# Moving the q and k loads behind the first head's one-hot copies in the SyncE queue, with the preparation steps shifted by one

## The reference

```
q_bits = einsum(q, proj) > 0 ; k_bits = einsum(k, proj) > 0          # 6 bits a row
mask   = bucket(q_bits)[:, :, :, None] == bucket(k_bits)[:, :, None, :]
scores = where(mask, q @ k.T / sqrt(D), -1e9)
attn   = exp(scores - max) / (sum + 1e-9)
x      = (attn @ v) as 1536 tokens x 512
h = x @ w_in1 ; g = (a0 + a1 h + a2 h^2 + a3 h^3) / (1 + |b0||h| + |b1|h^2 + 1e-6) ; x = g @ w_out1
h = x @ w_in2 ; g = h - tanh(h) ; out = g @ w_out2
```

## Time and profile before

| | us |
|---|---|
| median of 3 runs (750.47 to 751.36) | 751.3 |
| the profiled execution's own time | 751.21 |
| its span, first to last instruction | 749.4 |
| outside the span | 1.8 |
| attention, by PE's timeline | up to about 227 |

### The profile page before, as it was taken

How to read it: one execution, slowest core, us unless ns; L and a number is a source line. 1 busy time by engine, 2 the same in 40 slices (tenths; PEclk the granted TensorE clock), 3 DMA queues, 4 the chain that set the end, 5 groups by cost and what they waited for, 6 DMA issues and landing times.

```text
span 749.4 us, 11868 instructions
## 1 busy us (share of the span) xinstructions
PE 734.7 (98%) x3715; PEld 624.8 (83%) x3715; DVE 605.0 (81%) x931; ACT 484.1 (65%) x938; POOL 272.5 (36%) x249
## 2 busy tenths in 40 slices
PE   7998999999999999999999999999999999999998
PEld 4997998998998888788888888888888788888886
DVE  5987998888997999999988888975685698875622
ACT  7887888988897878788766867755553233322321
POOL 6685566566569000000000000000058499992000
PEclk9999999999999999999999999999999999999999
DMA  6758668768745500000000032320000110000101
GB/s 200 176 154 200 186 165 196 192 165 197 165 124 157 188 1 0 1 1 1 1 1 14 30 113 84 111 88 14 1 1 28 43 43 28 15 15 0 57 1 56
DMA packets 43612, 60.21 MB, mean 80 GB/s; under 512 B 7088, under 2 KB 25776, under 8 KB 43568
## 3 DMA queue, kind: packets, MB, share of 16 engines
q1 hardware_dynamic: 43424, 59.26, 29.3%
q10 hardware_dynamic: 144, 0.39, 0.1%
HBM read 31.66 MB, written 3.19 MB: 47 GB/s over the span
## 4 chain that ended last, share of the span: by engine, by line
PE 72%; DVE 10%; SPq 6%; POOL 5%; issue 4%; DMA 3%; ACT 1%; POOLq 0%; ACTq 0%; DVEq 0%
PE acc L867 31%; PE h_ps L833 18%; PE h_ps L957 9%; PE slot L266 5%; PE turn_ps L378 4%; PE pv_ps L342 2%; PE pv_ps L344 2%; DMA kA<-k_hot 2%; SPq L1388 2%; DVE sqr L1155 1%; DVE pol L1176 1%; SPq L1390 1%; DVE pol L1162 1%; SPq L1386 1%; DVE pol L1187 1%
## 5 line engine op out<-in xcount | busy, mean ns | idle before, releaser
L780 POOL TENSOR_TENSOR wout_raw<-win_hi 128x256 f32<-128x256 f32 x8 | 8.9, 1137 | 319.6 <-DVE win_lo L1208 309.2
L608 DVE TENSOR_TENSOR pt_lo<-turn_ps,pt_hi 128x384 fp32r<-128x384 f32 x192 | 97.8, 552 | 16.9 <-ACT pt_hi L522 16.6
L522 ACT ACTIVATE pt_hi<-turn_ps 128x384 fp32r<-128x384 f32 x192 | 85.2, 495 | 26.6 <-PE turn_ps L378 26.1
L833 PE MATMUL h_ps<-x_hi,win_lo 128*128 128x512 f32 x256 | 99.9, 390 | 0.0
L833 PE MATMUL h_ps<-x_lo,win_hi 128*128 128x512 f32 x256 | 99.6, 389 | 0.0
L833 PE MATMUL h_ps<-x_hi,win_hi 128*128 128x512 f32 x256 | 99.6, 389 | 0.0
L566 DVE TENSOR_REDUCE row_min<-slot 128x1 f32<-128x768 f32 x96 | 90.9, 948 | 5.8 <-PE slot L266 5.3
L996 ACT ACTIVATE g_hi<-pol 128x512 fp32r<-128x512 f32 x80 | 50.9, 637 | 66.5 <-PE acc L867 34.1
L454 ACT ACTIVATE E<-slot,row_min 128x768 f32<-128x768 f32 x96 | 87.4, 911 | 2.0 <-issue 1.7
L1200 DVE TENSOR_TENSOR g_lo<-pol,g_hi 128x512 fp32r<-128x512 f32 x80 | 65.9, 824 | 21.7 <-ACT g_hi L996 21.4
L378 PE MATMUL turn_ps<-ident,E 128*128 128x128 f32 x576 | 80.6, 274 | 0.4 <-DVE pt_lo L608 0.3
(11 more groups left out here) (192 smaller groups left out, 1811.4 us busy)
## 6 DMA issues: line engine op xcount, KB each, us to landing
win_raw<-in_moe_w_in SPq DMA_DIRECT2D x32, 256.0 KB, 3.3
wout_raw<-in_moe_w_out SPq DMA_DIRECT2D x32, 256.0 KB, 2.8
v_nat<-in_v SPq DMA_DIRECT2D x8, 384.0 KB, 4.1
q_t<-in_q SPq DMA_DIRECT2D x7, 384.0 KB, 3.1
k_t<-in_k SPq DMA_DIRECT2D x7, 384.0 KB, 3.7
qA<-q_hi SPq DMA_DIRECT2D x14, 192.0 KB, 3.7
qB<-q_hi SPq DMA_DIRECT2D x14, 192.0 KB, 4.0
qB<-q_lo SPq DMA_DIRECT2D x14, 192.0 KB, 4.1
```

The costliest lines, as they stand in the source:

```text
L522: eng.activation(pt_hi[:, c % 2, k0:k0 + T // 2, i * P:(i + 1) * P], turn_ps[h][:, 0:HALF].rearrange("r (k n) -> r k n", n=P), ACT.Copy).t ...
L608: eng.tensor_tensor(pt_lo[dst], turn_ps[h][:, 0:HALF].rearrange("r (k n) -> r k n", n=P), pt_hi[dst].bitcast(F32), ALU.subtract).then_inc( ...
L833: mm = eng.matmul(h_ps[t % 4][:, :], w[:, ws], columns(x, kt, c), start=kt + n == 0, stop=kt == KT - 1 and n == 2)
```

## The change

In SyncE's queue the loads of q and k of pair p + 2 go from the head of each pair's list to a place behind the one-hot copies of head 0 and the load of v, ahead of the split copies of head 1. The dots are taken in step 0 and the one-hots in steps 1 to 4 (they were in 1, and 2 to 5; in the first pair each is one step later than in the others). The sum of head 0 is taken in step 5 on ACT (it was 4), its reciprocal in step 6 on DVE (it was 5), and ACT scales q in step 9 (it was 8).

```diff
-        DOT_STEP = 1
-        HOT_STEPS = {2: (0, 0), 3: (1, 0), 4: (0, 1), 5: (1, 1)}
+        DOT_STEP = 0
+        HOT_STEPS = {1: (0, 0), 2: (1, 0), 3: (0, 1), 4: (1, 1)}
...
-                if first and n == 2:
-                    pe_dots(eng, 1)
-                if prepare and not first and n == DOT_STEP:
+                if prepare and n - first == DOT_STEP:
                     pe_dots(eng, p + 1)
...
-                if turn and n == 8:
+                if turn and n == 9:
                     act_scale(eng, p + 2)
...
-                if n in (4, 9 if last else 11):
+                if n in (5, 9 if last else 11):
                     act_sum(eng, p, n // T)
...
-                if n in (5, 9 if last else 11):
-                    dve_scale(eng, p, n // T)
+                if n in (6, 9 if last else 11):
+                    dve_scale(eng, p, int(n > T))
...
-                if first and n == 2:
-                    dve_bits(eng, 1)
-                if prepare and not first and n == DOT_STEP:
+                if prepare and n - first == DOT_STEP:
                     dve_bits(eng, p + 1)
...
                 def sync_att(p, turn=True):
-                    if turn:
-                        load_qk(p + 2, 0)
-                        load_qk(p + 2, 1)
                     copy_split(p + 1, 0)
                     if not is_zero(p):
                         shift(p - 1, 1)
                     scale_out(p, 0)
                     copy_hot(p + 1, 0)
                     load_v(p + 1)
+                    if turn:
+                        load_qk(p + 2, 0)
+                        load_qk(p + 2, 1)
                     copy_split(p + 1, 1)
```

## The result

The changed kernel takes 772.1 us (median of 5 runs, 769.8 to 776.2) against 751.4 us of the kernel before on the same chip: a ratio of 1.027, 95% interval 1.024 to 1.031, some 20.7 us slower. The profiled execution is the slowest of the five, 776.15 us with a span of 774.3, so that its terms add up to 4 us more than the median.

The account below looks back on a forecast made before the run. PE was taken to bound the kernel, busy 734.7 of 749.4 us. Idle time removed, new waits for q and slow clock sum as 751.2 - 7.1 + 15.8 + 4.4 = 764.3, so 764 us was predicted, range 752 to 773.

Parts of the forecast that it names:

- ACT waits for q in step 9 of six pairs, and PE in step 10: Pairs 0 to 5: q lands 4.3 us after issue, PE waits 2.64 us each, 15.8 us in all.
- v's situation: In SyncE's queue, q with v ahead and copies behind was likened to v, which landed in 4.4 and 5.1 us.
- The clock: Behind PE's new gaps: half of six lower the clock, 3 x 1.47 = 4.4 us lost to slow matmuls.
- the 7.1: PE idle time the change could remove in attention: 5.0 of copy waits, 1.47 of slow matmuls, 2 x 0.29 of scaling.
- The waits removed: PE's step 9 waits for head 0's last one-hot copy, 5.0 us in four places, go or nearly.
- The loop stays hidden: POOL, SyncE's queue and DMA: next q split 1.8 us later, hidden by a pair 2.6 us longer; otherwise next to bind.
- k at nothing: Dots in step 0 need k, landing about 4 us after issue, before the next pair begins; no cost.
- The reciprocal: Head 0's reciprocal, in step 6, gates `scale_out` in SyncE's queue, which is issued 2.5 us later than now.
- A load in time: Rival: q lands within 1.66 us of issue, PE sees no wait beyond 0.29 us for scaling; 745.8 us, chance 0.12.
- the short wait: Rival: q lands in 2.9 us, six waits of 1.24 us and no slow clock; 751.5 us, chance 0.18.
- The estimate from the Trainium skill's page: 2.0 us plus bytes at 436 GB/s: q takes 3.2 us from issue, the wait 1.5, total about 753 us; not followed.
- The long case: Rival: L = 5.1 or the loop binding too, all six gaps at low clock, 6 x (3.44 + 1.47); 773.6 us, chance 0.18.

Follow-up runs that it names:

- the queue experiment: The kernel before with only the two loads moved in SyncE's queue and ACT's scaling in step 9; 763.6 us, ratio 1.016.
- The run with v behind: The changed kernel with v's load issued behind the loads of q and k instead of ahead; 764.0 us, ratio 1.017.
- The filler run: The changed kernel with 14 unused matmuls ahead of PE's waiting scores of step 10 in pairs 0 to 5; 766.4 us, ratio 1.020.
- the half loads: The changed kernel, q and k loads of pairs 2 to 7 cut to 64 of 128 partitions: 754.2 us with scaling in step 11, 768.9 us in step 9.
- the experiment that only removed the first wait: The changed kernel with ACT scaling q in step 11 instead of 9, nothing else; 763.7 us, ratio 1.014.
- one-hot copies first: The kernel before, dots and one-hots a step earlier, head 0's one-hot copies directly behind its split copies, ahead of shift and `scale_out`; 755.7 us, ratio 1.005.
- copies held back: The changed kernel with SyncE waiting for q's landing before it issues the copies of head 1; 769.3 us, ratio 1.023.

## Why the prediction was right, and what in it was not
- **ACT waits for q in step 9 of six pairs, and PE in step 10.** Right, place by place, and the queue experiment shows it is the move of the loads that does it. q was issued when it was reckoned to be. The sizes: 4.3 us of landing was taken, 4.1 to 6.4 was measured, 5.1 on average and above my upper bound of 5.1 in three pairs. I called q's place v's situation, and it is not: v had only one-hot copies ahead, q has a whole load. The run with v behind shows what that is worth (3.1 to 3.5 us). PE's six waits were 18.8 us in the profile instead of 15.8.
- **The clock.** The term of 4.4 us was mis-sized most. I charged three of six gaps at 1.47 us. In the profile the clock fell with all five gaps of 2.26 us and more, and PE's busy time rose by 10.7. The kernel before had lost 1.47 of its own, which the forecast took out with the 7.1, so the term to set beside 4.4 is 12.2. The other four runs have a mean granted clock of 0.987 to 0.989 against 0.984 in the profiled one and lost a little less. The filler run gives 5.7 us in the median as the least part of it. The profiled execution lies 11.9 us above the sum: 7.8 are this term, 3.0 the waits, 0.4 the copy.
- **The waits removed.** 5.0 us of waits for the copy became 0.42, as said. That gain is real, but it is the shadow of the longer pair: with the new wait taken away it came back (10.4 us with the scaling in step 11, where the loop is longer than before).
- **The loop stays hidden.** Right: 0.4 us of PE's waits are for the copies. Its size was reckoned as 1.8 us a pair; the half loads give 1.6, but this has the clock and a wait for k in it, so the close match is in part luck. The sentence that it would bind next held too. What I left out is what it means for the cause: the two costs overlap, so neither has one price. With the loop long, taking the wait for q away gives back 8.4 us (772.1 to 763.7), and 12 us of loss stay. With half loads and so a shorter loop, the wait for q costs 14.7 us, and the kernel without it is 2.3 us slower than the one before. Four runs stop at 763.6 to 765.3 us, but not all for the loop: with the scaling in step 11 and with v behind PE's new waits are for one-hots and copies, while with the queue order alone and with the reciprocal in step 5 they are still for ACT.
- **k at nothing.** The dots in step 0 were taken to be covered, with k landing after about 4 us. It took 5.8 to 8.0 us in the changed kernel. The longer pair still covered that; with the scaling in step 11 the cover went once, for 2.0 us.
- **The reciprocal.** It was reckoned as the gate of the queue, and is: 7 us hang on it in the changed kernel.
- **The rivals.** A load in time (745.8 us) fell by ACT's six waits, the short wait (751.5 us) by their length and by the clock. The estimate from the Trainium skill's page "DMA: Bandwidth & Descriptors" (Anatomy of one DMA), about 753 us, is not borne out: q took 4.1 us at the least, against 3.2 by that page. The long case, 773.6 us, came nearest to the median; it got 0.18. Its mean landing time was right (5.1 us), its clock term of 8.8 us (six gaps at 1.47) still short of 12.2. The median of 772.1 us lies above the forecast's own range of 757 to 771 (its two allowances, 1.5 and 4 us, give no more than 758.5 to 769.5), and inside the whole range only because that took in most of the long case.

## What to carry to other kernels
A load that is moved down a queue is late by all that the queue waits for ahead of it, and shares the DMA engines with what is issued directly ahead of it and behind it: look for the first instruction that needs it, and for who is queued behind that one. When a wait is taken out, ask what is next: here a loop through the DMA queue had nearly the same period, so the experiment that only removed the first wait showed what the second is worth. Price each of two overlapping costs with the other one made small. Price an empty stretch of TensorE with the slow matmuls that follow it.

## What the runs showed of the hardware
- The same 384 KB load of q landed 2.9 to 3.4 us after its issue at the head of the queue (2.9 in the earlier trace rows), 3.1 to 3.5 us behind the one-hot copies with two loads behind it, and 4.1 to 6.4 us with v's load directly ahead. Half its bytes, in that last place, still took 4.2 to 4.5 us.
- What is issued behind a load can delay it: with the copies of head 1 held back, q landed in 3.7 to 4.6 us in pairs 1 to 5 instead of 4.2 to 6.4.
- The granted clock fell to 0.50 with every gap of 2.26 us and more in these traces. Between 1.78 and 2.21 us it went both ways: it fell after 1.78 and 1.82 us (one-hot copies first) and 1.96 (scaling in step 11), but not after 1.81 (loads at the head), 2.05 (scaling in step 11) or 2.21 (copies held back). In some cases it fell up to a microsecond after the matmuls had begun again. By the windows of the changed kernel it was low for 3.4 to 6.8 us each time (the missing share of each window's clock over one half); what of this PE was busy for ran at half the speed.
